# Two score passes in place of three for the second batch, one transpose in place of two

## The chip, the cores and the metric

The kernel runs on one core of one Trainium2 chip. The metric is the time in microseconds of one execution on the device; the median of several is compared. Engines are named as in the profile: PE is TensorE, PEld its weight loads, DVE is VectorE, ACT is ScalarE, POOL is GpSimd, SP is SyncE, which here only starts DMAs.

## The reference

```python
# attention: B=2, H=8, S=768, D=64, n_sink=4, window=128
scores = q @ k.T / sqrt(D)
keep = (key < 4) | ((query - key >= 0) & (query - key < 128))
a = softmax(where(keep, scores, -1e9))           # denominators + 1e-9
x = concat_heads(a @ v)                          # (2, 768, 512)
# first mixer
u = x + (x.T @ U @ V).T                          # U (768, 32), V (32, 768)
x = u + relu(u @ w_ch1) @ w_ch2                  # 512 -> 2048 -> 512
# second mixer
u = x + (relu(x.T @ w_tok1) @ w_tok2).T          # 768 -> 256 -> 768
out = u + relu(u @ w_ch1) @ w_ch2                # 512 -> 1536 -> 512
```

## The kernel before

**Number format.** Matrices are multiplied in float32r, TensorE's faster form of float32 with fewer bits. To keep precision each operand is split into a high part (the rounded value) and a low part (the rest), and a product is made of three matmul passes: high by high, high by low, low by high. ScalarE or VectorE writes high parts, VectorE or GpSimd subtracts to get low ones (`w_lo = w_raw - w_hi`, line 786).

**Attention.** Queries are cut into 12 tiles of 128 (`T`, six a batch); a head of a tile is a unit `u = 8 T + h`, from 0 to 95. The window of 128 means that a tile needs only its own keys and those of the tile before, besides the 4 sinks: 264 columns of scores, two blocks of 132. Three key tiles are kept in `k_hi` and `k_lo`. The array's 128 rows hold two heads of 64 channels. Each head's keys stand in its own half of the rows with zeros in the other half, so that the queries of a pair of heads can be the weights of both.

A unit goes as follows. TensorE makes the three score passes (L1264). VectorE adds the mask and takes the minimum of the negated scores (L1012). ScalarE makes the exponentials `probs` and their sum (L839). GpSimd copies the sink columns, already weighted, to `p_sink` (L751). TensorE transposes the two 128x128 blocks of probabilities (L1272, float32) into the bank `tp_banks`, which it shares with the transposes of q and k (L1249). ScalarE (odd units) or VectorE (even units) copies them to `probs_T` (L848, L1023). TensorE multiplies with v (L1292, float32, which the trace shows as two records a block). In a tile's last unit the sinks are transposed and multiplied (L1280, L1301), and VectorE scales the sum into `x_nat` (L1037).

In the window of a tile, own keys are kept for key <= query, those of the tile before for key > query. So the two blocks' kept entries never lie at the same place. The masked ones are zeros after the exponential.

**The plan.** One list of steps, `plan`, is built up front; every engine walks it and issues its own part of each step, in this order. Waits are semaphores. The first batch's attention runs alone, a head after the other. The second batch's (units 48 to 95) is strewn between the products of the first batch's first mixer: after every `mm1` (12 matmuls, L1413) or `mm2` (9 matmuls, L1448) one unit follows. There the transposes of unit u stand in unit u+2 and its product with v in unit u+3. Transposes of the next tile's q come in the unit h = 0, those of k and the split of q in h = 3, the splits of k (`ksplit`, `ksplit_odd`) in h = 5 and h = 7. In the first batch they stand at h = 0, 2, 4 and 6, and the lags are 2 and 4.

ScalarE copies q and k out of the bank into `q_full`, `k_full` (L815, L822), VectorE makes `q_hi` and `k_hi` (L972, L990), GpSimd `q_lo` and `k_lo` (L511, L522).

**Weights.** Each of mm1, mm2 uses one chunk of 128x512. SP loads it up to 6 ahead, ScalarE writes `w_hi` (L807) and GpSimd `w_lo` (L786) for the third chunk ahead, into rings of 4.

**The other places that the change touches.** The step `up` of layer 1, batch 0 leaves its result in four banks. ScalarE and VectorE split it into `uT_hi`, `uT_lo` (L795, L952), a quarter `kk` for each. mm1 with f = 0 begins with a wait for the last quarter, and its 12 matmuls take the quarters in turn, three each.

After this the other three mixers (layer 1 batch 1, layer 2 batches 0 and 1) use seven products of half size in place of eight (`s1`, `s2`, L1229), whose sums VectorE builds out of banks (L1132, L1135, L1138) and of which ScalarE copies the first (L924). Before each, the operands' sums are split on ScalarE (L903) and VectorE (`b_lo`, L1106). At the end of an `mm2` series in layer 2, VectorE copies the three finished output tiles to `o_stage` (L1182), and SP stores them.

## Time and profile before

| | us |
|---|---|
| median of 3 runs | 646.53 (646.51 to 646.6) |
| the profiled execution | 646.83 |
| its span, first to last instruction | 645.0 |
| TensorE busy | 628.4 (97%) |
| VectorE, ScalarE, GpSimd busy | 344.2, 323.0, 371.7 |

The profile is of one execution. Matmuls are pipelined: their records overlap, so what a matmul costs in a stream is the distance from its start to the next one's, not its duration. The first batch's attention ends at about 73 us; the units of the second lie between 73 and 237 us; the last three mixers follow.

### The profile page before, as it was taken

The numbers are of one execution on the slowest core, as the hardware profiler recorded it, in microseconds if no ns is written. First come the engines' busy times: TensorE is split into PE (matmuls) and PEld (weight loads), VectorE is DVE, ScalarE is ACT, GpSimd is POOL, SyncE is SP. The second block draws the span as 40 slices with busy tenths as digits, with TensorE's granted clock in tenths as the row PEclk, the third lists the DMA queues.
The fourth block names the chain that finished last, engine by engine and source line by source line (L and its number), as shares of the span: only waits on it lengthen the run. The fifth ranks groups of instructions, "written<-read, shape, count | busy, mean of one in ns | idle before, by whom it ended". The sixth has DMA issues, their size and how long they took to land.

```text
span 645.0 us, 10417 instructions
## 1 busy us (share of the span) xinstructions
PE 628.4 (97%) x3554; PEld 566.7 (88%) x3554; DVE 344.2 (53%) x728; ACT 323.0 (50%) x731; POOL 371.7 (58%) x371
## 2 busy tenths in 40 slices
PE   7999899999999999999999999999999999999997
PEld 6889698999999997999999988899998888899986
DVE  7776643332343336675775741396578227675411
ACT  5657655545454455745444444555444446444321
POOL 8545456655656475467566554676656446567262
PEclk9999999999999999999999999999999999999999
DMA  7434343442333324322323342433323343431142
GB/s 171 117 85 121 79 115 94 126 125 82 99 100 112 117 68 145 99 99 66 115 82 81 100 121 76 113 102 97 91 91 113 100 144 84 138 93 33 50 145 83
DMA packets 88468, 65.61 MB, mean 102 GB/s; under 512 B 43040, under 2 KB 72480, under 8 KB 88416
## 3 DMA queue, kind: packets, MB, share of 16 engines
q1 hardware_dynamic: 88416, 64.95, 35.6%
q8 instruction: 29, 0.48, 0.3%
q14 instruction: 23, 0.19, 0.1%
HBM read 61.52 MB, written 3.15 MB: 100 GB/s over the span
## 4 chain that ended last, share of the span: by engine, by line
PE 86%; DVE 7%; ACT 2%; issue 2%; POOL 1%; DMA 0%; DVEq 0%; ACTq 0%; POOLq 0%
PE bank L1448 32%; PE bank L1229 22%; PE bank L1413 10%; PE bank L1292 4%; PE bank L1264 4%; PE bank L1377 3%; PE bank L1272 3%; PE bank L1339 3%; PE bank L1249 1%; DVE b_lo L1106 1%; PE bank L1353 1%; PE bank L1320 1%; PE bank L1440 1%; DVE masked L1012 1%; POOL w_lo L786 1%
## 5 line engine op out<-in xcount | busy, mean ns | idle before, releaser
L786 POOL TENSOR_TENSOR w_lo<-w_raw,w_hi 128x512 fp32r<-128x512 f32 (+1 forms) x158 | 209.6, 1332 | 154.1 <-ACT w_hi L807 153.6
L807 ACT ACTIVATE w_hi<-w_raw 128x512 fp32r<-128x512 f32 (+1 forms) x158 | 96.8, 618 | 55.1 <-PE bank L1448 37.1
L1229 PE MATMUL bank<-b_hi,a_hi 128*128 128x384 f32 x280 | 94.7, 338 | 1.6 <-DVE temps L1135 1.5
L1229 PE MATMUL bank<-b_lo,a_hi 128*128 128x384 f32 x280 | 94.8, 338 | 0.0
L1448 PE MATMUL bank<-w_hi,hid_hi 128*128 128x512 f32 x216 | 86.8, 402 | 0.3 <-DVE hid_lo L949 0.3
L1448 PE MATMUL bank<-w_hi,hid_lo 128*128 128x512 f32 x216 | 85.1, 394 | 0.0
L1448 PE MATMUL bank<-w_lo,hid_hi 128*128 128x512 f32 x216 | 84.7, 392 | 0.0
L839 ACT ACTIVATE probs<-masked,neg_max 128x264 f32<-128x264 f32 x96 | 49.5, 516 | 69.8 <-DVE neg_max L1012 69.1
L1448 PE MATMUL bank<-w_hi,y_hid 128*128 128x512 f32 x216 | 71.1, 394 | 0.2
L1012 DVE CUSTOM_DVE_ANT_0 masked<-bank,masks 128x264 f32<-128x264 f32 x96 | 41.1, 430 | 40.0 <-PE bank L1264 36.8
L751 POOL COPY p_sink<-probs 128x12 f32<-128x12 f32 x96 | 20.3, 213 | 70.2 <-ACT probs L839 68.7
L1229 PEld LDWEIGHTS bank<-b_hi,a_hi 128*128 128x128 f32 x280 | 52.6, 188 | 3.7 <-issue 1.8
L1229 PEld LDWEIGHTS bank<-b_lo,a_hi 128*128 128x128 f32 x280 | 52.7, 188 | 1.6
L1292 PE MATMUL bank<-v_nat,probs_T 128*128 128x64 f32 x352 | 50.3, 261 | 1.3 <-DVE probs_T L1023 1.0
L949 DVE SCALAR_TENSOR_TENSOR hid_lo<-bank,hid_hi 128x384 fp32r<-128x384 f32 x32 | 17.8, 557 | 62.0 <-ACT hid_hi L795 62.0
L1292 PEld LDWEIGHTS bank<-v_nat,probs_T 128*128 128x128 f32 x352 | 48.1, 190 | 3.1 <-DVE probs_T L1023 1.4
L1448 PEld LDWEIGHTS bank<-w_hi,y_hid 128*128 128x128 f32 x216 | 40.5, 188 | 9.5 <-POOL w_lo L786 1.5
L1448 PEld LDWEIGHTS bank<-w_hi,hid_lo 128*128 128x128 f32 x216 | 40.5, 188 | 9.0
L1229 PE MATMUL bank<-b_hi,a_lo_even 128*128 128x384 f32 x140 | 47.3, 338 | 0.0
L1229 PE MATMUL bank<-b_hi,a_lo_odd 128*128 128x384 f32 x140 | 47.1, 336 | 0.0
L1413 PE MATMUL bank<-uT_hi,w_hi 128*128 128x384 f32 x128 | 45.3, 354 | 1.6 <-DVE uT_lo L952 1.6
L1448 PEld LDWEIGHTS bank<-w_hi,hid_hi 128*128 128x128 f32 x216 | 40.6, 188 | 7.0 <-issue 0.7
(157 smaller groups left out, 1423.3 us busy)
## 6 DMA issues: line engine op xcount, KB each, us to landing
w_raw<-in_moe_w_ch_dram SPq DMA_DIRECT2D x144, 256.0 KB, 2.7
w_raw<-in_moe_w_ch_dram SPq DMA_DIRECT2D x20, 512.0 KB, 3.5
q_nat<-in_q_dram SPq DMA_DIRECT2D x12, 256.0 KB, 3.0
k_nat<-in_k_dram SPq DMA_DIRECT2D x12, 256.0 KB, 3.5
v_nat<-in_v_dram SPq DMA_DIRECT2D x12, 256.0 KB, 3.5
out_dram<-o_stage SPq DMA_DIRECT2D x11, 256.0 KB, 3.4
w_raw<-in_moe_w_tok_dram SPq DMA_DIRECT2D x6, 256.0 KB, 2.7
w_raw<-in_moe_w_tok_dram SPq DMA_DIRECT2D x8, 192.0 KB, 2.4
```

What stands on the lines that cost most here:

```text
L751: nc.gpsimd.tensor_copy(p_sink[:, T % 2, :].rearrange("p (c n) -> p c n", c=3)[:, :, N_SINK * h:N_SINK * (h + 1)], probs[:, u % 4, P:BLK]. ...
L786: nc.gpsimd.tensor_tensor(w_lo[:, split % NW, 0:n], w_raw[:, split % NR, 0:n], w_hi[:, split % NW, 0:n].bitcast(f32), ALU.subtract) \
L807: nc.scalar.activation(w_hi[:, split % NW, 0:n], w_raw[:, split % NR, 0:n], ACT.Copy) \
L839: nc.scalar.activation(probs[:, u % 4, :], masked[:, u % 3, :], ACT.Exp, bias=neg_max[:, u % (2 * H):u % (2 * H) + 1], scale=-1.0, accum_o ...
L1012: nc.vector.tensor_tensor_reduce(out=masked[:, u % 3, :], in0=s_slots(u)[0][:, 0:NK], in1=masks[:, mask_of(T), :], scale=1.0, scalar=3.0e3 ...
L1229: last = mm(bank[:, 0:HALF], w[at % 2][:, a, k, :], u[:, b_part, k, :], start=(first and n == 0), stop=(n == 5), skip_group_check=True)
L1264: last = mm(bank[:, 0:NK], qs[:, T % 2, h // 2, :], keys(ks, T, h // 2, h % 2), start=(n == 0), stop=(n == 2))
L1272: last = nc.tensor.transpose(tp_banks[tp_bank_of[s]][:, j * P:(j + 1) * P], probs[:, u % 4, col:col + P], ident[:, :])
L1292: last = mm(o_bank(T)[:, h * D:(h + 1) * D], probs_T[:, u % 2, j * P:(j + 1) * P], v_nat[:, tile % 3, h * D:(h + 1) * D], start=(h == 0 an ...
L1339: last = mm(m_tile(use)[:, :], w[:, slot, cols], x[:, t % 2, :], start=(t == 0 and n == 0), stop=(t == NQ - 1 and n == 2), skip_group_chec ...
L1413: last = mm(m_tile(use)[:, 0:HALF], w[:, slot, rows], u[:, kk, cols], start=(n == 0), stop=(n == 3 * KD - 1))
L1448: last = mm(m_tile(use)[:, :], stationary, w[:, slot, :], start=False, stop=(final and n == 2), skip_group_check=True)
```

## The change

1. **Scores of the second batch (T >= 6) in two passes.** A new tile `q_both` holds, for head e of a pair, the low queries in the head's own half of the rows and its high queries in the other half. `k_hi` now holds the head's high keys in both halves, where one half was zero. One pass over `q_both` and `k_hi` gives low by high plus high by high. The second is high by `k_lo`, whose other half is still zero.
2. **What fills them.** VectorE copies the high queries to the other half (two operations of 64 rows, `q_moved`), GpSimd makes the low ones in two operations of 64 rows in place of one of 128, ScalarE copies the high keys to the other half (two operations of 64 rows, `k_moved`), and the sinks' columns once (`ksinks`).
3. **One transpose (T >= 7, 40 units).** GpSimd adds the second block of probabilities to the first. TensorE transposes the one sum. VectorE multiplies the transposed sum with two triangles of ones and gets both blocks of `probs_T`, for odd units too. The triangles are built once on GpSimd, in `o_stage`, at the step `("pv", 8)`.
4. **Output tiles of layer 2, batch 0, second half** are copied to `o_stage` by ScalarE in place of VectorE.
5. **mm1 with f = 0** waits for the quarters of `up` one after the other, each ahead of its three matmuls.
6. One buffer's name and place in memory change (`a_hi_odd` stands where a 32-column filler was).

```diff
@@ blocks
+            if T > NQ:
+                return [(0, T), (0, T - 1)]
@@ query_low(eng, wait, T)
+            if T >= NQ:
+                for e in range(2):
+                    rows = slice(e * D, (e + 1) * D)
+                    wait(q_split, queries_split(T - 1) + e)
+                    eng.tensor_tensor(q_both[rows, T % 2, :, e, :], q_full[rows],
+                                      q_hi[rows, T % 2, :, :].bitcast(f32), ALU.subtract).then_inc(q_split, 1)
+                wait(q_split, queries_split(T))
+                return
@@
+        def two_triangles(T):
+            return T > NQ
         def by_act(u):
-            return u % 2 == 1
+            return u % 2 == 1 and not two_triangles(u // H)
+        def copied_by_act(s):
+            return s[:4] == ("mm2", 2, 0, 1)
@@ gpsimd, scores
+                    if two_triangles(T):
+                        pool.wait_ge(probs_ready, u + 1)
+                        nc.gpsimd.tensor_tensor(probs[:, u % 4, 0:P], probs[:, u % 4, 0:P],
+                                                probs[:, u % 4, BLK:BLK + P], ALU.add).then_inc(blocks_added, 1)
@@ gpsimd, qsplit
                     pool.wait_ge(q_high, s[1] + 1)
+                    pool.wait_ge(psink_ready, copied)
+                    if split:
+                        pool.wait_ge(wlo_ready, split)
@@ gpsimd
+                elif s == ("pv", H):
+                    nc.gpsimd.memset(triangles[:, :, :], 1.0).then_inc(triangles_built, 1)
...
@@ scalar
+                elif s[0] == "ksplit" and s[1] >= NQ:
+                    T = s[1]
+                    act.wait_ge(k_copied, T + 1)
+                    act.wait_ge(scores_ready, H * (T - 1))
+                    for e in range(2):
+                        src = list(key_parts(k_hi, T))[e][0]
+                        last = nc.scalar.activation(k_hi[(1 - e) * D:(2 - e) * D, :, e, T % 3, 0:P], src, ACT.Copy)
+                    last.then_inc(k_moved, 1)
...
@@ scalar, sinksT
+                    if two_triangles(T):
+                        wait_drained(act, ("probsT", H * T + H - 1))
@@ scalar
+                elif copied_by_act(s) and ends(s):
+                    for i in range(TPH):
+                        act.wait_ge(m_ready, m_at[s[:4], i] + 1)
+                        act.wait_ge(out_stored[i], 16)
+                        nc.scalar.activation(o_stage[:, i, :], m_tile((s[:4], i))[:, :], ACT.Copy).then_inc(y_copied, 1)
@@ vector, qsplit
+                    if T >= NQ:
+                        for e in range(2):
+                            rows, there = slice(e * D, (e + 1) * D), slice((1 - e) * D, (2 - e) * D)
+                            moved = nc.vector.tensor_copy(q_both[there, T % 2, :, e, :], q_full[rows])
+                        moved.then_inc(q_moved, 1)
@@ vector, probsT
+                    if two_triangles(u // H):
+                        dve.wait_ge(triangles_built, 3)
+                        nc.vector.tensor_tensor(probs_T[:, u % 2, :].rearrange("p (a b) -> p a b", a=2),
+                                                transposed[:, 0:P].unsqueeze(1).broadcast_to([P, 2, P]),
+                                                triangles[:, :, :], ALU.mult).then_inc(probsT_by_dve, 1)
@@ tensor, scores
-                    for n, (qs, ks) in enumerate(((q_hi, k_hi), (q_hi, k_lo), (q_lo, k_hi))):
+                    if T < NQ:
+                        passes = ((high, k_hi), (high, k_lo), (low, k_hi))
+                    else:
+                        passes = ((q_both[:, T % 2, h // 2, h % 2, :], k_hi), (high, k_lo))
@@ tensor, probsT
                     pe.wait_ge(probs_ready, u + 1)
                     tp_free(s)
+                    if two_triangles(u // H):
+                        pe.wait_ge(blocks_added, u - (NQ + 1) * H + 1)
@@ tensor, mm1
-                    if f == 0:
-                        wait_out((("up", layer, b, half), KD - 1))
...
                     for kk in range(KD):
                         rows = slice(kk * P, (kk + 1) * P)
+                        if f == 0:
+                            wait_out((("up", layer, b, half), kk))
```

## Rows read from the trace of the kernel before

**Rows 1.** The page: busy time, share and instructions; the chain by engine.
```profile
PE 628.4 (97%) x3554; PEld 566.7 (88%) x3554; DVE 344.2 (53%) x728; ACT 323.0 (50%) x731; POOL 371.7 (58%) x371
...
PE 86%; DVE 7%; ACT 2%; issue 2%; POOL 1%; DMA 0%; DVEq 0%; ACTq 0%; POOLq 0%
```

**Rows 2.** Windows: stretch, its length, busy us of each engine, granted clock, DMA.
```profile
79.00:91.00 12.00, 10.14 (x62) 9.28 (x61) 6.28 (x19) 6.88 (x18) 4.83 (x7) 1.00 0.50 136
...
130.00:157.00 27.00, 26.85 (x172) 24.90 (x172) 8.99 (x30) 13.53 (x36) 16.33 (x20) 1.00 0.39 108
```

**Rows 3.** Timeline of one unit: start us, duration us, engine, instruction.
```profile
182.94 0.28 PE L1264 MATMUL bank<-k_hi,q_hi 128*128 128x264 f32 x1
...
183.18 0.29 PE L1264 MATMUL bank<-k_hi,q_lo 128*128 128x264 f32 x1
...
183.30 0.55 PE L1292 MATMUL bank<-v_nat,probs_T 128*128 128x64 f32 x4
...
183.69 0.39 PE L1272 MATMUL bank<-ident,probs 128*128 128x128 f32 x2
...
183.92 0.27 PE L1280 MATMUL bank<-ident,p_sink 128*96 128x128 f32 x1
...
184.65 0.19 POOL L751 COPY p_sink<-probs 128x12 f32<-128x12 f32 x1 [1.32 <-ACT probs L839]
```

**Rows 4.** Timeline of a unit that begins with the transposes of k.
```profile
163.74 0.60 ACT L822 ACTIVATE uT_full<-bank 128x512 f32<-128x512 f32 x1 [1.24 <-PE bank L1249]
...
163.84 0.55 PE L1292 MATMUL bank<-v_nat,probs_T 128*128 128x64 f32 x4
...
164.48 0.41 PE L1272 MATMUL bank<-ident,probs 128*128 128x128 f32 x2
```

**Rows 5.** Timeline ahead of the first mm1.
```profile
78.87 1.95 DVE L952 TENSOR_TENSOR uT_lo<-bank,uT_hi 128x384 fp32r<-128x384 f32 x4 [1.05 <-ACT uT_hi L795]
...
80.88 0.44 PE L1413 MATMUL bank<-uT_hi,w_hi 128*128 128x384 f32 x1 [1.56 <-DVE uT_lo L952]
...
81.09 0.29 DVE L1023 COPY probs_T<-bank 128x128 f32<-128x128 f32 x1
```

**Rows 6.** Timeline of the last mixer's first products.
```profile
542.36 1.14 ACT L807 ACTIVATE w_hi<-w_raw 128x512 fp32r<-128x512 f32 x2
...
543.05 3.50 POOL L786 TENSOR_TENSOR w_lo<-w_raw,w_hi 128x512 fp32r<-128x512 f32 x2 [0.45 <-ACT w_hi L807]
...
547.28 1.87 DVE L1182 COPY o_stage<-bank 128x512 f32<-128x512 f32 x3
...
548.53 0.33 PE L1229 MATMUL bank<-b_hi,a_lo_even 128*128 128x384 f32 x1
...
549.65 0.56 DVE L1135 TENSOR_TENSOR temps<-bank,temps 128x384 f32<-128x384 f32 x1
...
550.36 0.41 PE L1229 MATMUL bank<-b_hi,a_hi 128*128 128x384 f32 x1 [1.50 <-DVE temps L1135]
```

**Rows 7.** Groups by form, whole span: count, busy us, mean ns of one, idle before.
```profile
L786 POOL TENSOR_TENSOR w_lo<-w_raw,w_hi 128x512 fp32r<-128x512 f32 x150 | 201.5, 1348 | 144.0 <-ACT w_hi L807 143.6
...
L522 POOL TENSOR_TENSOR k_lo<-uT_full,k_hi 64x512 fp32r<-64x512 f32 x22 | 28.4, 1291 | 6.2 <-DVE k_hi L990 2.4 <-POOL w_lo L786 2.0 <-POOL p_sink L751 0.3
...
L1023 DVE COPY probs_T<-bank 128x256 f32<-128x256 f32 x40 | 16.9, 422 | 7.6 <-PE bank L1272 7.3
...
L511 POOL TENSOR_TENSOR q_lo<-uT_full,q_hi 128x512 fp32r<-128x512 f32 x11 | 14.1, 1282 | 2.7 <-DVE q_hi L972 2.7
...
L990 DVE CAST k_hi<-uT_full 64x512 fp32r<-64x512 f32 x22 | 11.0, 498 | 0.2
...
L786 POOL TENSOR_TENSOR w_lo<-w_raw,w_hi 128x384 fp32r<-128x384 f32 x8 | 8.2, 1035 | 10.0 <-ACT w_hi L807 10.0
```

**Rows 8.** Timeline: ScalarE where tile 6 is prepared, VectorE's casts of tile 7.
```profile
65.18 0.52 ACT L839 ACTIVATE probs<-masked,neg_max 128x264 f32<-128x264 f32 x1 [0.72 <-DVE neg_max L1012]
...
90.46 1.84 DVE L990 CAST k_hi<-uT_full 64x512 fp32r<-64x512 f32 x2
```

More of the change, by code:

```diff
@@ L362, in attention_then_two_mixers @@
         temps = sb("temps", [P, 3, HALF])
-        sb("above_probs", [P, 32])
+        a_hi_odd = sb("a_hi_odd", [P, 7, 2, P], f32r)
         w1_sums = sb("w1_sums", [P, 3, 2, P])
         w1_raw = sb("w1_raw", [P, 2, KD, 2 * P])
-        a_hi = [sb(f"a_hi{i}", [P, 7, 2, P], f32r) for i in range(2)]
+        a_hi = [sb("a_hi_even", [P, 7, 2, P], f32r), a_hi_odd]
         a_lo = [sb("a_lo_even", [P, 7, 2, P], f32r), a_lo_odd]
@@ L507, in by_pair, with queries_split, query_low @@
             return bank[:, :].rearrange("p (a b) -> p a b", a=PAIRS)
-        def query_low(eng, T):
+        def queries_split(T):
+            return T + 1 if T < NQ else 2 * (T + 1) - NQ
+        def query_low(eng, wait, T):
+            if T >= NQ:
[6 more added lines that the diff above has]
+                return
             eng.tensor_tensor(q_lo[:, T % 2, :, :], q_full,
@@ L540, in o_bank, with act_copies @@
             return o_banks[T % 2] if T < NQ else o_banks[0]
+        def two_triangles(T):
+            return T > NQ
         def by_act(u):
-            return u % 2 == 1
+            return u % 2 == 1 and not two_triangles(u // H)
+        def act_copies(u):
+            return sum(by_act(v) for v in range(u + 1))
         def wait_drained(eng, s):
@@ L584, in attention_then_two_mixers @@
         for key in m_at:
-            if y1_at(key) is None and not (key[0][0] == "up" and key[0][1:3] in SEVEN):
+            if y1_at(key) is None and not copied_by_act(key[0]) and not (key[0][0] == "up" and key[0][1:3] in SEVEN):
                 drained_at[key] = len(drained_at)
@@ L1166, in _ @@
                     low_of((s, 0), every, hid_lo[:, hid_slot(s), :], hid_hi[:, hid_slot(s), :], relu=True)
+                elif copied_by_act(s):
+                    stored += TPH if ends(s) else 0
                 elif s[0] == "mm2" and ends(s):
@@ L1262, in _ @@
                         pe.wait_ge(masked_ready, u - n + 1)
-                    for n, (qs, ks) in enumerate(((q_hi, k_hi), (q_hi, k_lo), (q_lo, k_hi))):
-                        last = mm(bank[:, 0:NK], qs[:, T % 2, h // 2, :], keys(ks, T, h // 2, h % 2),
-                                  start=(n == 0), stop=(n == 2))
+                    high, low = q_hi[:, T % 2, h // 2, :], q_lo[:, T % 2, h // 2, :]
+                    if T < NQ:
+                        passes = ((high, k_hi), (high, k_lo), (low, k_hi))
+                    else:
+                        passes = ((q_both[:, T % 2, h // 2, h % 2, :], k_hi), (high, k_lo))
+                    for n, (queries, ks) in enumerate(passes):
+                        last = mm(bank[:, 0:NK], queries, keys(ks, T, h // 2, h % 2),
+                                  start=(n == 0), stop=(n == len(passes) - 1))
                     last.then_inc(scores_ready, 1)
@@ L1270, in _ @@
                     tp_free(s)
-                    for j, (col, _) in enumerate(blocks(u // H)):
+                    if two_triangles(u // H):
+                        pe.wait_ge(blocks_added, u - (NQ + 1) * H + 1)
+                    for j, (col, _) in enumerate(blocks(u // H)[0:1 if two_triangles(u // H) else 2]):
                         last = nc.tensor.transpose(tp_banks[tp_bank_of[s]][:, j * P:(j + 1) * P],
```

56 lines of the change are left out of this document (44 added, 12 removed).

## The prediction

> **What bounds the kernel now.** I read the page first: TensorE is busy 97% of the span, and 86% of the chain that ended last is its work [rows 1]. A busy share can hide stalls, so I next cut the changed stretch, from 79 us (where the second batch's heads lie between the first mixer's products) to 233 us, into windows. From 130 to 157 us, eight heads, TensorE is busy 26.85 of 27 at a granted clock of 1.00 (2.4 GHz), while VectorE, ScalarE and GpSimd have 9.0, 13.5 and 16.3 us of work. Only the first window, 79 to 91 us, has a hole, 10.14 of 12 [rows 2]. So work taken from TensorE there shortens the span, as long as nobody else falls behind. Last I read the timeline at one head and at the two places where other edits lie.
>
> **The score passes.** One head's first pass starts at 182.94, its third at 183.18, the next work at 183.30 [rows 3]: 0.12 us a pass. One pass goes in each of 48 heads: 48 x 0.12 = 5.8 us. The pass over stacked rows has the same shape as the one it replaces, so it costs the same. The Trainium skill (TensorE: Matmul & The Clock Gate, Back-to-back issue gap) gives N/2.4 + 2.5 ns, 112 ns here, an estimate by which this term is 5.4; the row decides.
>
> **The transposes.** For tiles 7 to 11 (40 heads) one of two goes. Two start at 183.69 and the next transpose, of the same length, at 183.92 [rows 3]: 0.115 each. 40 x 0.115 = 4.6, and with the change of kind behind them nearer 4.8, which I take; bounds 4.6 and 5.2 (0.13 each). The same page and section has about 81 ns a matmul at N = 128 in a stream, an estimate of 3.2 us for this term; these are float32 transposes and the trace is slower than that, so the trace's number stands.
>
> **What the shorter head gives back.** Where a head begins with the transposes of q or k, the next probability transpose needs the same bank, which ScalarE first has to copy out. At 163.74 ScalarE copies for 0.60, TensorE's four p.v matmuls start at 163.84 and the transpose at 164.48 [rows 4]. The four take 0.39 elsewhere (183.30 to 183.69) [rows 3], so 0.25 us are a wait. It hangs on the copy, not on the passes, so a pass removed ahead of it only lengthens it. There are nine such heads (q for tiles 8 to 11, k for 7 to 11): -9 x 0.12 = -1.1 us.
>
> **The wait by quarters before the first mm1.** TensorE is idle 1.56 us until 80.88, for VectorE's four uT_lo subtractions that begin at 78.87 and take 1.95 [rows 5]. It needs only the first quarter to begin: ready at about 78.87 + 0.55 = 79.4. A quarter's three matmuls last 0.53, a subtraction 0.49, so each later quarter is ready when wanted. Start at 79.5 instead of 80.88: 1.4, less a little for breaking the stream of weight loads: 1.3 us. What is next late is the bank of the following k transposes, which holds until VectorE has copied out head 48's probabilities at 81.4 [rows 5]; the product now ends near 81.7, so it just fits. Bounds: 0.7 (if this and the tile's masks bite) to 1.4. The same edit at the second half finds its quarters long drained: nothing.
>
> **The output copies moved to ScalarE.** At 547.28 VectorE comes from a series of b_lo subtractions to copy three output tiles (1.87 us), and only then makes the next mixer's sums, the second at 549.65; TensorE stands 1.50 idle until 550.36 for it [rows 6]. Without the copies the two sums (0.56 each) run from 547.4 to 548.5. TensorE's last matmul before the hole begins at 548.53 and the next one would begin 0.18 later, at 548.7: nearly all of 550.36 - 548.7 = 1.65 comes back. ScalarE takes the three copies at 0.6 each (a 128x512 copy out of a bank [rows 4]) from 543.5, when its two w_hi end [rows 6], to 545.3. Behind them is its copy of the first product, half a microsecond, which VectorE wants at 547.4. Its three a_hi come a microsecond later too, and their user GpSimd is busy with w_lo until 546.55 [rows 6]. The stores, issued on SP some steps into the next mixer, find the tiles ready as before. I take 1.6; bounds 0.8 to 1.7.
>
> **What is added, and its cover.** *GpSimd.* The add of two 128x128 blocks is not in the trace. Its two-input operation takes 1348 ns for 512 columns and 1035 for 384 [rows 7], 2.45 ns a column, which leaves 0.41 us for 128. From below it is bounded by the 12-column p_sink copy, 0.19 [rows 3], from above by the full 512-column operation, 1.35. I take 0.41, which the slope of two rows supports. The q_lo of a tile becomes two operations on half the rows; k_lo shows that half the rows cost the same, 1291 against 1282 ns [rows 7]: +1.29 us a tile. In 130 to 157 us GpSimd was busy 16.33 of 27 [rows 2]; it becomes 16.33 + 1.29 + 8 x 0.41 = 20.9, in 27 - 8 x 0.24 = 25.1. It stays under. Behind the add on its queue are p_sink, then w_lo for the third chunk ahead, which has some two steps of 3 us in hand, and the next tile's q_lo and k_lo. TensorE now waits for the add: probabilities of a head are ready about 1.7 us after its passes begin (182.94 to the p_sink copy at 184.65 [rows 3]), and their transpose comes two heads later, some 6 us after. Even behind two q_lo's (2.6) and a w_lo (1.3) the add keeps the date. Cost 0; if that cover goes, see the rivals.
> *VectorE.* The product with the triangles replaces a copy out of the same bank, 422 ns [rows 7], and has as many columns; it may cost up to the 384-column sum out of a bank, 0.56 [rows 6]. It takes over ScalarE's 20 copies. With the two q moves (0.50 each, as its k_hi cast [rows 7]) that is 4 x 0.42 + 1.0 = 2.7 us more in a tile, at most 4.3, on 9 of 27 busy [rows 2]. Hidden; what waits behind is the mask of the head, which TensorE wants only at the next head's passes, 3 us on.
> *ScalarE.* Two k moves of at most 0.6 in (half the rows of the copy in [rows 4]), four copies of some 0.4 out: even.
> *At the border of the batches* cover is thinner, since heads follow each other in 1.2 us. Tile 6's preparation adds 1.2 us to ScalarE just ahead of a probability that runs at 65.18 after 0.72 idle [rows 8]: that one comes half a microsecond late, and is used four heads on. GpSimd gets a second q_lo there and, in the first batch, the triangles (three small operations, together under one q_lo); head 48 waits for two small moves more. I charge 0.4 for all of this; bounds 0 and, if each of the two ScalarE moves and the q_lo comes through, 2.5.
>
> **Sum.** 5.8 + 4.8 - 1.1 + 1.3 + 1.6 - 0.4 = 12.0 us. The profiled execution took 646.83; the span is 645.0, with 1.8 around it, unchanged. 646.83 - 12.0 = 634.8. The median before, 646.53, is 0.3 lower than that execution, so the median should be about 634.5, which I predict.
>
> **Rivals.**
> *A, only removed matmuls pay.* The 1.56 and 1.50 us holes move instead of closing: head 48's bank and masks are late after the first, the b_lo series rules after the second. For it: both are chains through VectorE, and 81.4 against 81.7 is close. Against: in both the next thing is ready by the rows. Time: 646.5 - (5.8 + 4.8 - 1.1 - 0.4) = 637.4.
> *B, GpSimd late in some heads.* Its two-input operations stretch when VectorE works beside: two w_lo's took 3.50 beside b_lo [rows 6], and two k_hi casts 1.84 in place of 1.0 [rows 8]. New VectorE moves come exactly when the two q_lo's run. If the transposes of the three heads a tile with q_lo or k_lo work (15) wait 0.3 us each, that is 4.5 back: 639. The Trainium skill (GPSIMD Engine Reference, Engine selection) says to put elementwise two-input work on VectorE and not here, and in Key points that the two share SBUF interfaces; the stretched rows agree with the sharing. Against: over 3 us of slack.
> *C, slower: GpSimd becomes the bound.* Between tiles 7 and 11 every head needs its add. From an add of (25.1 - 17.6)/8 = 0.94 us on, GpSimd has no idle time and sets the pace; at 1.35, the price of the full 512 columns, eight heads take 17.6 + 10.8 = 28.4 instead of 27: 5 x 1.4 = 7 us lost, against 2.9 gained at the two holes and 1 in tile 6: 650. For it: half the rows cost as much as all, so size isn't everything here. Against: the slope over columns.
> *D, the passes pay less than their spacing*, because a hidden limit (weight loads are busy 24.9 of 27 us [rows 2]) steps in: half of 10.6 less: 640.
>
> **How the numbers follow.** Forecast 0.73, A 0.12, B 0.07, C 0.03, D 0.05. Added bounds of the terms put the forecast between 646.5 - (5.8 + 5.2 - 1.1 + 1.4 + 1.7) = 633.5 and 646.5 - (5.8 + 4.6 - 1.1 + 0.7 + 0.8 - 2.5) = 638.2; A's 637.4 lies inside. The range is 632.9 to 638.6: it leaves B, C and D out, and takes in that half of the 1.1 is not given back. What can be told from no change is about 0.2%, 1.3 us: faster 0.95, same 0.02, slower 0.03, of which the slower is C.
>
> **What would show it.** Right: 48 score passes and 40 transposes fewer; heads 0.24 us shorter; the first mm1 starting near 79.5; no hole of over 0.3 us among the first products of the last mixer; an add of some 0.4 us; GpSimd near 83% in the middle windows. Wrong: TensorE idle until the add at a transpose (B, C), a hole of the same size moved a few matmuls on (A), or passes spaced wider than 0.12 us (D).

## The result, and the profile after

The changed kernel takes **638.50 us** (median of 4 runs, 638.29 to 638.59) against 646.57 (646.51 to 646.72) for the kernel before, run beside it: ratio 0.9874, 95% interval 0.9857 to 0.9892. That is 8.1 us faster where 12.0 had been forecast, and 0.1 inside the upper end of the range (638.6). The profiled execution took 638.47, of which the span is 636.4.

What an execution takes beyond its span isn't the same for all kernels: 1.8 us for the kernel before, 2.1 for the changed one and for e1, e5 and e7 below, 1.7 for e4 and e12, and it varies by about 1 us between executions of e6 and of e8. The profile doesn't say what it is. So the medians of two kernels can lie 0.3 to 0.4 us closer or further apart than their spans.

The page of the kernel after, the lines that answer to [rows 1]: 88 matmuls fewer, as many as the change takes out.

```profile
PE 619.0 (97%) x3466; PEld 556.3 (87%) x3466; DVE 360.0 (57%) x757; ACT 326.5 (51%) x728; POOL 396.8 (62%) x420
...
PE 85%; DVE 8%; issue 3%; ACT 2%; POOL 1%; DMA 0%; DVEq 0%; ACTq 0%; POOLq 0%
```

TensorE's busy time fell by 9.4 us (628.4 to 619.0), the span by 8.6. The same windows as [rows 2]:

```profile
79.00:91.00 12.00, 10.23 (x59) 8.94 (x60) 7.67 (x18) 6.33 (x18) 6.75 (x7) 1.00 0.51 132
130.00:157.00 27.00, 26.65 (x167) 24.64 (x166) 14.73 (x40) 14.88 (x39) 21.27 (x31) 1.00 0.45 120
```

In the middle of the tiles it went as forecast: TensorE nearly full, GpSimd at 21.3 of 27 us. In the first window it did not: of the 1.56 us hole of [rows 5] 0.39 is left, and TensorE has still as little work done, 10.23 of 12. Something else opened there. VectorE got more work than the bound allowed. The products take 0.42 in each of a tile's eight heads in place of four, and the two q moves take 3.0: 4.7 us more in a tile in the middle, where "at most 4.3" stood, a bound whose terms the text doesn't give.

The groups of instructions between 79 and 233 us, by form (count, busy us, mean ns of one, idle before), show the price of what was added:

```profile
L786 POOL TENSOR_TENSOR probs<-probs 128x128 f32<-128x128 f32 x40 | 19.4, 484 | 21.3 <-ACT probs L908 19.7 <-POOL q_both L528 0.4
L1108 DVE TENSOR_TENSOR probs_T<-bank,o_stage 128x256 f32<-128x256 f32 x40 | 16.8, 421 | 2.5 <-PE bank L1374 1.1 <-PE bank L1382 0.5
...
L1052 DVE CAST q_both<-uT_full 64x512 fp32r<-64x512 f32 x10 | 12.8, 1276 | 0.2
```

The add takes 0.48 us (0.41 was taken), the product with the triangles 0.42 (as taken). A q move on VectorE takes 1.28 us where 0.50 had been taken.

**How to find where time went.** For two kernels with the same order of work I subtract the start of the same matmul: the second score pass (k_lo, q_hi) of each head, and the first product with b_hi, a_hi of each step of the mixers. I call the difference the lead over before. Heads are counted from 0; head 48 is the first of tile 6. The leads, in us, of the kernels that the text below needs most (e9, e10 and so on are the names of the runs below):

| lead at | head 50 | 51 | 53 | 55 | 95 | mixer (1,1) begins | last mixer, before its sums | after them | last product |
|---|---|---|---|---|---|---|---|---|---|
| after | -0.97 | +0.36 | -1.23 | -1.01 | 6.27 | 5.69 | 6.58 | 8.42 | 8.66 |
| only the transposes (e4) | -0.24 | 1.09 | 0.96 | 0.96 | 4.77 | 5.10 | 5.97 | 7.81 | 8.05 |
| q moves on ScalarE (e9) | -1.08 | 0.25 | 0.23 | -0.53 | 6.19 | 5.61 | 6.22 | 8.01 | 8.25 |
| q, k transposes inside (e10) | -0.69 | 0.34 | -1.16 | -0.95 | 7.46 | 6.88 | 7.71 | 9.48 | 9.72 |
| both of these (e11) | -0.83 | 0.19 | 0.42 | -0.35 | 8.43 | 7.85 | 8.46 | 10.26 | 10.49 |
| only the transposes, inside (e12) | -0.14 | 0.91 | 1.01 | 1.02 | 5.99 | 6.31 | 7.14 | 8.91 | 9.15 |

In the row "after" 0.7 us are lost at the border of the batches, ahead of head 50 (0.26 of the -0.97 is there from the start of the kernel). The quarter wait gives 1.33 at head 51; 1.6 us are lost again by head 53; then 7.3 us come in over the 40 heads from 55 to 95; 0.6 are lost before the mixer (1,1); 1.8 come at the last mixer's sums.

**Where the 1.6 us went** is seen in the timeline of the kernel after, 84 to 90 us:

```profile
84.97 1.84 DVE L1052 CAST q_both<-uT_full 64x512 fp32r<-64x512 f32 x2
...
85.02 2.94 POOL L528 TENSOR_TENSOR q_both<-uT_full,q_hi 64x512 fp32r<-64x512 f32 x2 [0.36 <-DVE q_hi L1048]
...
86.85 0.43 DVE L1093 CUSTOM_DVE_ANT_0 masked<-bank,masks 128x264 f32<-128x264 f32 x1
...
87.32 0.52 ACT L908 ACTIVATE probs<-masked,neg_max 128x264 f32<-128x264 f32 x1 [3.16 <-DVE neg_max L1093]
...
87.84 0.26 ACT L917 ACTIVATE probs_T<-bank 128x128 f32<-128x128 f32 x1
87.99 0.48 ACT L846 ACTIVATE uT_hi<-bank 128x384 fp32r<-128x384 f32 x1
...
88.15 0.43 PE L1394 MATMUL bank<-v_nat,probs_T 128*128 128x64 f32 x2 [0.29 <-ACT probs_T L917]
...
88.50 0.56 DVE L1028 TENSOR_TENSOR uT_lo<-bank,uT_hi 128x384 fp32r<-128x384 f32 x1 [1.22 <-ACT uT_hi L846]
...
89.12 0.55 PE L1455 MATMUL bank<-ident,x_nat 128*128 128x128 f32 x3 [0.42 <-DVE uT_lo L1028]
```

Start at 88.15. TensorE waits there for probabilities that ScalarE copied at 87.84. Their transpose was done since 84.6; but in ScalarE's order the copy stands behind the exponential of the next head (87.32), which waits for VectorE's mask (86.85), which stands behind the two q moves (84.97). So a move that TensorE needs 16 us later (tile 7's first pass starts at 101.26) delays by 1.8 us a copy that is needed now. ScalarE was idle 3.16 us ahead of it.

The larger wait is one link further down the same queue. Behind the copy ScalarE splits `uT_hi` (87.99), from it VectorE makes `uT_lo` (88.50), and TensorE waits for that at 89.12. From the product with v to these next transposes it is 0.97 us, where it was 0.28 before. The late mask itself shifts the score passes of head 52 by another 0.3.

**The border of the batches**, in the timeline from 62 to 69 us: the q moves of tile 6 (0.43 each here), then VectorE's k_hi casts of the same tile, ScalarE's new k moves, and who waits.

```profile
62.76 0.86 DVE L1052 CAST q_both<-uT_full 64x512 fp32r<-64x512 f32 x2
...
65.59 1.26 DVE L1071 CAST k_hi<-uT_full 64x512 fp32r<-64x512 f32 x2
...
66.61 1.27 ACT L891 ACTIVATE k_hi<-uT_full 64x512 fp32r<-64x512 f32 x2
...
67.48 0.69 DVE L1125 TENSOR_TENSOR x_nat<-bank,recip 128x512 f32<-128x512 f32 x1
...
68.23 0.67 PE L1422 MATMUL bank<-x_nat,U_sb 128*96 128x512 f32 x1 [0.70 <-DVE x_nat L1125]
```

VectorE is late with the tile's output: before, its q_hi cast ended at 62.46 with 0.65 us to spare before the mask, the k_hi casts took 0.85 and not 1.26, and TensorE waited 0.14 us for x_nat; now it waits 0.70.

**A new hole of 0.91 us behind the heads**, in the timeline from 226 to 241 us:

```profile
226.97 0.46 POOL L786 TENSOR_TENSOR probs<-probs 128x128 f32<-128x128 f32 x1 [0.63 <-ACT probs L908]
...
233.07 5.05 POOL L837 TENSOR_TENSOR w_lo<-w_raw,w_hi 128x512 fp32r<-128x512 f32 x4
...
236.85 1.43 DVE L1143 TENSOR_TENSOR b_hi<-U_sb,b_hi 128x128 fp32r<-128x128 f32 x1 [0.44 <-ACT b_hi L936]
...
238.34 2.38 DVE L1148 TENSOR_TENSOR b_lo<-x_nat,b_hi 128x512 fp32r<-128x512 f32 x2
...
238.63 1.53 POOL L837 TENSOR_TENSOR w_lo<-w_raw,w_hi 128x512 fp32r<-128x512 f32 x1 [0.51 <-ACT w_hi L858]
...
240.86 0.47 PE L1415 MATMUL bank<-b_hi 128*128 128x512 f32 x1 [0.91 <-DVE b_lo L1148]
```

The same two b_lo took 1.28 us in the kernel before. Here GpSimd's w_lo begins ahead of the second one, and they take 2.38. The lead falls from 6.73 at the first product with these operands to 5.69 behind them: 1.0 us. The change doesn't touch these operations; e6 below shows what shifted them.

**The last mixer**, the answer to [rows 6]. ScalarE copies the tiles at 536.82, VectorE goes from its b_lo straight to the sums, and the stream of products has no hole as in [rows 6]:

```profile
536.82 1.55 ACT L994 ACTIVATE o_stage<-bank 128x512 f32<-128x512 f32 x3
...
540.70 0.55 DVE L1220 TENSOR_TENSOR temps<-bank,temps 128x384 f32<-128x384 f32 x1
541.28 0.56 DVE L1223 TENSOR_TENSOR temps<-bank,temps 128x384 f32<-128x384 f32 x1
```

### The profile page after: what moved, and what is told of

Same layout as the page of the kernel before. It is cut to its first block, busy times and chain, and to the rows that moved or that the text cites. A ratio compares the mean times of both kernels' runs of the same rounds, so it can differ in the third digit from the quotient of the medians.

```text
span 636.4 us, 10351 instructions
## 1 busy us (share of the span) xinstructions
PE 619.0 (97%) x3466; PEld 556.3 (87%) x3466; DVE 360.0 (57%) x757; ACT 326.5 (51%) x728; POOL 396.8 (62%) x420
## 4 chain that ended last, share of the span: by engine, by line
PE 85%; DVE 8%; issue 3%; ACT 2%; POOL 1%; DMA 0%; DVEq 0%; ACTq 0%; POOLq 0%
PE bank L1550 33%; PE bank L1321 23%; PE bank L1515 9%; PE bank L1394 4%; PE bank L1364 3%; PE bank L1479 3%; PE bank L1441 3%; PE bank L1374 2%; PE bank L1341 1%; DVE b_lo L1194 1%; PE bank L1455 1%; DVE masked L1093 1%; PE bank L1422 1%; PE bank L1542 1%; DVE b_lo L1148 1%
## 5 line engine op out<-in xcount | busy, mean ns | idle before, releaser
L1321 PE MATMUL bank<-b_hi,a_hi_even 128*128 128x384 f32 x140 | 47.1, 336 | 0.1
L1321 PE MATMUL bank<-b_hi,a_hi_odd 128*128 128x384 f32 x140 | 46.9, 335 | 0.0
L1321 PE MATMUL bank<-b_lo,a_hi_odd 128*128 128x384 f32 x140 | 46.9, 335 | 0.0
L1321 PE MATMUL bank<-b_lo,a_hi_even 128*128 128x384 f32 x140 | 46.9, 335 | 0.0
L1550 PEld LDWEIGHTS bank<-w_lo,hid_hi 128*128 128x128 f32 x216 | 40.6, 188 | 6.7
```

The costliest lines, as they stand in the source:

```text
L1321: last = mm(bank[:, 0:HALF], w[at % 2][:, a, k, :], u[:, b_part, k, :], start=(first and n == 0), stop=(n == 5), skip_group_check=True)
L1550: last = mm(m_tile(use)[:, :], stationary, w[:, slot, :], start=False, stop=(final and n == 2), skip_group_check=True)
```

## The experiments

All were timed beside the kernel before. The theory that I had formed from the traces (M in the expectations): each part pays what it was said to pay where it stands, and the missing 4 us are handed back at places where VectorE or ScalarE, not TensorE, sets the pace. Its rivals: H, a shift of the engines against each other accounts for the loss; D, the passes pay less than their spacing; B, GpSimd is late. From e9 on the rival is R: work taken from one late engine only makes the next one late.

### One wait in place of four (e1)

```diff
+                    if f == 0:
+                        wait_out((("up", layer, b, half), KD - 1))
...
-                        if f == 0:
-                            wait_out((("up", layer, b, half), kk))
```

> The changed kernel, with the first mm1 waiting once, for the last quarter, as before the change. Theory M (late masks: VectorE's moves of q hold the mask of head 51 back, and with it the probabilities, and that chain begins only when mm1 has ended, so it follows mm1 wherever it lies): the 1.3 us that the quarters brought are lost again, 639.8. Rival H (the hole only moved: mm1 ends too early for what follows it, and heads 52 and 53 pay 1.6 us for that): nothing changes, 638.3 to 638.6.

Measured 639.29 (638.99 to 640.31), ratio 0.9885 (0.9872 to 0.9899). That lies between M's 639.8 and H's 638.6 at most. The hole is back:

```profile
81.55 0.44 PE L1515 MATMUL bank<-uT_hi,w_hi 128*128 128x384 f32 x1 [1.69 <-DVE uT_lo L1028]
```

Its lead at head 50 is -0.68 where after has -0.97: 0.29 that the two have apart since their first microseconds. Beyond that it is 1.33 behind after at head 51, 0.75 at head 53, and 1.04 at the end (lead 7.91); the medians differ by 0.8. So the wait by quarters gains 1.3 where it stands, as forecast. By head 53 0.6 of it is handed back, and at the end 0.3; the medians say 0.5.

### The output copies on VectorE again (e2)

```diff
-            return s[:4] == ("mm2", 2, 0, 1)
+            return False
```

> The changed kernel, with the output tiles of layer 2, batch 0, second half copied by VectorE again. In the changed trace the hole of 1.5 us is gone; both theories expect it back: 638.5 + 1.6 = 640.1. Should other work take its place, 638.5.

Measured 641.13 (640.25 to 641.97), ratio 0.9906 (0.9891 to 0.9921). The lead behind the sums is 6.47 in place of 8.42: this part is worth 1.95 us there, where 1.6 had been expected. The medians are 2.6 apart, and the four executions are spread over 1.7 us. In the profiled one another 1.1 us lie behind the last product (4.9 us to the end of the span, 3.8 in after), where the output is stored; nothing here tells why. The timeline has the sequence of [rows 6] again:

```profile
540.85 1.87 DVE L1272 COPY o_stage<-bank 128x512 f32<-128x512 f32 x3
...
543.93 0.41 PE L1321 MATMUL bank<-b_hi,a_hi_even 128*128 128x384 f32 x1 [1.50 <-DVE temps L1223]
```

### The two halves of the change alone (e3, e4)

e3, two transposes again, passes as changed:

```diff
-            return T > NQ
+            return False
...
-            if T > NQ:
-                return [(0, T), (0, T - 1)]
```

> The changed kernel with two transposes a head and no add and no triangle product in tiles 7 to 11 (score passes stay two). Theory M: 40 transposes come back at 0.12 us each, 638.5 + 4.8 = 643.3; ScalarE has its 20 copies again, and they stand behind exponentials that late masks delay, which costs up to 1 us more. Rival D (removed matmuls pay half their spacing): 638.5 + 2.4 = 640.9.

Measured 643.26 (642.4 to 643.54), ratio 0.9941 (0.9929 to 0.9954). M had 643.3. Its lead at the last product is 3.99, so taking one transpose in place of two is worth 4.7 us on top of the passes, near the forecast. But other things are mixed into this number. Over heads 55 to 95 after gains 5.3 us on e3, more than the transposes' own spacing gives (37 of them, 0.115 each: 4.3), because e3 has ScalarE copy probabilities again, and these copies stand behind the exponentials that the q moves delay:

```profile
115.32 0.66 PE L1392 MATMUL bank<-v_nat,probs_T 128*128 128x64 f32 x4 [0.26 <-ACT probs_T L915]
```

Behind the heads after loses 1.0 of it in the b_lo hole, which e3 doesn't have.

e4, one transpose, three passes as before, nothing held twice:

```diff
-                        if T >= NQ:
-                            pe.wait_ge(q_moved, T - NQ + 1)
-                            pe.wait_ge(k_moved, T - NQ + 2)
...
-                    if T < NQ:
+                    if True:
                         passes = ((high, k_hi), (high, k_lo), (low, k_hi))
```

(with all moves and the second q_lo left out)

> The changed kernel with three score passes and without all that fills the stacked rows (no moves of q and k, one q_lo of 128 rows); transposes stay one a head. Theory M: +5.8 us of passes, -0.7 us at the border and -1.6 us at heads 52 and 53, which the preparation causes: 642.0. Rival D: passes pay half, +2.9 - 2.3: 639.1. Rival H: preparation costs nothing at heads 52 and 53, +5.8 - 0.7: 643.6.

Measured **638.61** (638.38 to 638.99), ratio 0.9873 (0.9859 to 0.9886): as fast as the whole change. M had 642.0, H 643.6; D's 639.1 is the closest (e5 answers it). The half of the change that stands first in its name, 48 passes fewer, is worth next to nothing on balance: 0.1 us by the medians, 0.6 by the leads. Row "only the transposes" of the table says where it went. By head 55 it leads after by 1.97, though it has run seven passes more (0.84): the preparation costs 2.8. Over the next 40 heads after gains 3.5 on it, where 40 x 0.12 are 4.8: another 1.3 gone. And it has no b_lo hole (1.0). 5.8 - 2.8 - 1.3 - 1.0 leaves 0.7; the leads at the end differ by 0.6.

### The third pass back, the preparation kept (e5)

```diff
-                        passes = ((q_both[:, T % 2, h // 2, h % 2, :], k_hi), (high, k_lo))
+                        passes = ((q_both[:, T % 2, h // 2, h % 2, :], k_hi), (high, k_lo), (high, k_lo))
```

It adds one product twice; only the time counts.

> The changed kernel with the second score pass of the second batch made twice, so that TensorE has its 48 passes back while all preparation stays as changed (the scores come out wrong by one low term; only the time is read). Theory M: 48 x 0.12 = 5.8 us less what the nine heads with q or k transposes swallow, 1.1: 643.2. Rival D (a pass pays half its spacing): 641.1.

Measured 641.44 (641.18 to 641.75), ratio 0.9916 (0.9901 to 0.9932). M had 643.2, D 641.1. 48 passes cost 2.9 us here, not 5.8. The leads divide it: up to head 55 they cost 0.4 of 0.84, over heads 55 to 95 3.5 of 4.8 (the rest falls into waits), and the b_lo hole isn't there, which gives 1.0 back. D's number is close, its mechanism isn't there: in after the passes of a head stand at 95.12 and 95.24, the next work at 95.36, and the lead grows by 0.22 to 0.24 a head wherever no wait follows.

### No add on GpSimd (e6)

The add of the two probability blocks and TensorE's wait for it are left out, so half of each window is missing from the output; only the time counts.

```diff
-                    if two_triangles(T):
-                        pool.wait_ge(probs_ready, u + 1)
-                        nc.gpsimd.tensor_tensor(probs[:, u % 4, 0:P], probs[:, u % 4, 0:P],
-                                                probs[:, u % 4, BLK:BLK + P], ALU.add).then_inc(blocks_added, 1)
```

> The changed kernel without GpSimd's add and without the wait for it: the first block of probabilities alone is transposed (attention over half the window; only the time is read). Theory M: the add is never waited for, 638.5, or 0.2 less since GpSimd leaves VectorE's moves more room. Rival B (GpSimd late): up to 2 us faster, 636.5.

Measured 637.79 (637.22 to 638.61), ratio 0.9856 (0.9835 to 0.9877). M had 638.5 or 0.2 less, B 636.5. In the heads the leads are those of after within 0.2; TensorE never waited for the add. What it gains, 0.7 by the medians and 0.9 by the leads, comes at one place: the b_lo hole isn't there.

```profile
236.93 1.01 DVE L1139 TENSOR_TENSOR b_hi<-U_sb,b_hi 128x128 fp32r<-128x128 f32 x1 [0.44 <-ACT b_hi L932]
...
238.00 1.28 DVE L1144 TENSOR_TENSOR b_lo<-x_nat,b_hi 128x512 fp32r<-128x512 f32 x2
...
238.72 1.71 POOL L833 TENSOR_TENSOR w_lo<-w_raw,w_hi 128x512 fp32r<-128x512 f32 x1 [0.93 <-ACT w_hi L854]
```

The two traces, laid over each other at the first product with b_hi (239.32 in after, 239.40 in e6), show the steps. In after the last head's add (226.97) stands ahead of GpSimd's weight work, which then runs without a pause and ends 1.20 us before that product (238.12). In e6 it ends 1.61 before (237.79). VectorE's b_hi subtraction runs beside it and takes 1.43 us in place of 1.01, so VectorE's second b_lo starts 0.4 later. In e6 it starts 0.1 ahead of GpSimd's next w_lo and takes 0.68; in after 0.3 behind it, and takes 1.78. The next w_lo itself starts 0.69 before the product in both. The traces of all kernels agree: the hole is in the eight that have both the add and two passes (after, e1, e2, e7 to e11) and in none of the six that lack one or both (before, e3 to e6, e12). So B falls for the heads, but GpSimd is late by 0.4 us at their end, and that, through VectorE, costs 1.0.

### The q moves elsewhere (e7, e8, e9)

If the q moves at 84.97 are the cause, they must be put where nobody waits. Three tries. e7, still on VectorE, in the same head of the tile before as in after, but behind its mask and not ahead of it:

```diff
+                    if NQ <= N < NTILES and u % H == (2 if T < NQ else 3):
+                        for e in range(2):
+                            ...
+                            moved = nc.vector.tensor_copy(q_both[there, N % 2, :, e, :], q_full[rows])
```

> The changed kernel with VectorE's two q moves behind the mask of the same head in place of ahead of it. Theory M: the late masks go, and with them most of the 0.7 us at the border and of the 1.6 us at heads 52 and 53: 636.7. The moves still take up to 3 us a tile beside GpSimd, so what stands behind them on VectorE (the copy of probabilities) is late instead, hence not all. Rival H: 638.5.

Measured 640.70 (640.61 to 640.98), ratio 0.9905 (0.989 to 0.992): 2.2 slower than after, where M had 636.7. Timeline and windows at the border of the batches:

```profile
63.68 2.54 DVE L1097 CAST q_both<-uT_full 64x512 fp32r<-64x512 f32 x2
66.14 0.41 DVE L1113 COPY probs_T<-bank 128x256 f32<-128x256 f32 x1
...
66.70 0.41 PE L1375 MATMUL bank<-ident,probs 128*128 128x128 f32 x2 [1.89 <-DVE probs_T L1113]
```

```profile
64.00:68.00 4.00, 2.11 (x17) 1.92 (x15) 3.91 (x8) 1.17 (x7) 2.13 (x3) 0.94 0.86 195
68.00:72.00 4.00, 4.00 (x20) 3.46 (x20) 2.03 (x8) 3.06 (x8) 2.73 (x5) 0.64 0.01 4
```

The two casts took 2.54 in place of 0.86, and TensorE stood 1.89 idle; behind that its granted clock is 0.64 of full on average over 4 us. At heads 52 and 53 the mask is no longer late, but 1.15 us are lost all the same (1.59 in after): the two moves take 2.70 us at 87.75, and now `uT_lo` stands behind them.

e8, the q moves and the k moves on ScalarE, behind exponentials of the tile before:

```diff
+                    if NQ <= N < NTILES and h == (3 if T < NQ else 4):
+                        ...
+                            last = nc.scalar.activation(q_both[there, N % 2, :, e, :], q_full[rows], ACT.Copy)
+                    if NQ <= N < NTILES and h == (4 if T < NQ else 5):
+                        ...
+                            last = nc.scalar.activation(k_hi[(1 - e) * D:(2 - e) * D, :, e, N % 3, 0:P], src, ACT.Copy)
```

> The changed kernel with the q moves on ScalarE, behind an exponential one head later, and the k moves behind that head's exponential too. Theory M: ScalarE does not share GpSimd's way to the memory, a move takes 0.63 us there, and no mask waits: the whole 2.3 us come back, 636.2. Rival H: 638.5 less 0.7 at the border, 637.8.

Measured 640.74 (639.9 to 641.54), ratio 0.9905 (0.9889 to 0.9922), where M had 636.2. The gain and a new loss both happened. The lead at head 53 is +0.30 in place of -1.23: the 1.5 us came back. Then the k moves did two heads later what the q moves had done, on the other engine:

```profile
94.55 1.27 ACT L916 ACTIVATE k_hi<-uT_full 64x512 fp32r<-64x512 f32 x2
95.72 0.26 ACT L924 ACTIVATE probs_T<-bank 128x128 f32<-128x128 f32 x1
...
96.03 0.43 PE L1396 MATMUL bank<-v_nat,probs_T 128*128 128x64 f32 x2 [1.58 <-ACT probs_T L924]
...
98.43 0.63 PE L1552 MATMUL bank<-w_hi,hid_hi 128*128 128x512 f32 x1
98.86 0.63 PE L1552 MATMUL bank<-w_lo,hid_hi 128*128 128x512 f32 x1
```

The matmuls of 512 columns follow each other in 0.43 us instead of 0.23 until 99.7. This trace is of the slowest of the five executions (641.54, mean clock 0.997). Another has 0.997 too; the three others have a mean clock of 1.00 and spans of 637.9 to 638.2, 1.5 to 1.8 above after's. So the hole costs about its own length, and the slow stretch behind it comes in some executions only.

e9, only the q moves on ScalarE; the k moves stay:

> The q moves on ScalarE, two heads ahead of the tile, as in the run before; the k moves stay where the change has them. M (the two casts of the q move on VectorE, 1.84 us beside GpSimd's q_lo at 84.97, are what hands back the gain at head 52; and the hole of 1.58 us at 96.03 in the run before came from the k moves, that stood ahead of ScalarE's copy of the probabilities): the 1.5 us of head 52 come back and the hole doesn't: 637.0 (636.6 to 637.6). R (the work is only pushed to the next late engine): 638.2 to 638.8, with a new wait behind the exponential that the moves now follow.

Measured 638.50 (638.09 to 638.62), ratio 0.9868 (0.9853 to 0.9883). At head 53 the lead is +0.23, 1.46 more than after, and the chain is as M has it:

```profile
84.97 0.42 DVE L1096 CUSTOM_DVE_ANT_0 masked<-bank,masks 128x264 f32<-128x264 f32 x1
...
87.42 0.33 PE L1397 MATMUL bank<-v_nat,probs_T 128*128 128x64 f32 x2
```

But the time is that of after; M had 637.0, R 638.2 to 638.8. Of the 1.46 us, 0.98 are gone at head 55 (the tile's k_hi casts, 1.85 us, now come in time to be waited for: 0.18 for a mask, 0.29 for ScalarE's copy), 0.3 at head 57 (the wait for uT_full grows from 0.45 to 0.72), 0.5 at head 86; some 0.35 come back between. M is right about the cause at head 52, and R about what it is worth.

### The q and k transposes inside the product ahead (e10), and with the q moves on ScalarE (e11)

The wait named under "what the shorter head gives back" is [rows 4] again; in after, the timeline of the same unit:

```profile
160.95 0.60 PE L1341 MATMUL bank<-ident,k_nat 128*128 128x128 f32 x4
...
161.63 0.55 PE L1394 MATMUL bank<-v_nat,probs_T 128*128 128x64 f32 x4
...
161.67 0.60 ACT L877 ACTIVATE uT_full<-bank 128x512 f32<-128x512 f32 x1 [1.04 <-PE bank L1341]
...
162.37 0.30 PE L1374 MATMUL bank<-ident,probs 128*128 128x128 f32 x1 [0.18 <-issue]
162.51 0.41 PE L1515 MATMUL bank<-uT_hi,w_hi 128*128 128x384 f32 x1
```

From k's transposes to the probability transpose it is 1.42 us (1.44 before) though a pass less lies between. The edit moves the transposes and ScalarE's copy forward:

```diff
+                        if kk == 2 and s in next_tp:
+                            nat_transposes(next_tp[s])
...
+                        if i == 1 and s in next_tp:
+                            nat_transposes(next_tp[s])
... (scalar)
+                if s in next_tp:
+                    copy_nat(next_tp[s])
```

> The transposes of a tile's queries and keys, and ScalarE's copies of them, are put inside the product of the first batch ahead of them, ahead of its last third, in place of behind it. M (at the nine heads with such transposes the shorter passes only lengthen the wait for ScalarE's uT_full copy, 0.3 to 0.6 us each): the copy is under way before the probabilities are asked for: 9 x 0.3 to 0.4 = 3 us: 635.5 (634.8 to 636.5). R (the wait is for ScalarE's queue, and other copies come late instead): 638 to 639.

Measured 637.59 (637.4 to 638.53), ratio 0.986 (0.9843 to 0.9876). M had 635.5, R 638 to 639. A gain of 0.9, of which the heads behind q's transposes (57, 65, 73, 81) show 0.4 to 0.5 each. At those behind k's the 0.4 to 0.6 gained (60, 68, 76) are lost one head earlier (0.6 to 0.7 at 59, 67, 75), where TensorE now waits for VectorE to leave the bank, and another 0.5 goes from head 84 to 87:

```profile
158.92 0.41 DVE L1119 TENSOR_TENSOR probs_T<-bank,o_stage 128x256 f32<-128x256 f32 x1
...
159.48 0.63 PE L1348 MATMUL bank<-ident,k_nat 128*128 128x128 f32 x4 [0.38 <-DVE probs_T L1119]
```

> Both edits of the two runs ahead. If their gains are independent, their sum: 638.5 - 1.5 - 3.0 = 634.0. If one eats the other: the better of the two, 635.5.

Measured **636.49** (636.26 to 636.56), ratio 0.9837 (0.9823 to 0.9852): the fastest, 2.0 under after. The q moves on ScalarE, worth nothing alone, are worth 1.1 us on top of e10 by the medians and 0.8 by the leads. M's sum had 634.0 or, if one eats the other, 635.5.

### Only the transposes, with those inside (e12)

e4 and e10 together.

> The transposes' half of the change alone (three passes, no moves, as in the earlier run of 638.61), with the q and k transposes inside the product ahead. M (the passes' 5.8 us are eaten in part by the wait at those heads, in part by the moves and the b_lo split): with neither of these in the way the passes are worth what is left over; this kernel keeps the wait-free heads but not the passes: 638.6 less 9 x 0.2 = 636.8, so that the kernel with both edits beats it by 2.8 us. R (the score passes' half is worth nothing however it is prepared): as fast as the kernel with both edits, within 0.6 us.

Measured 637.49 (637.3 to 637.62), ratio 0.9853 (0.9838 to 0.9868). Against e11 it is 1.0 us slower by the medians, 1.3 by the leads. So the score passes' half of the change is worth 1.0 to 1.3 us when it is prepared better, and 0.1 to 0.6 as it was made: neither 2.8 (M) nor nothing (R, within 0.6).

## Why the prediction was right, and where it was not

The sign, the order of size and most terms held; one term, the cover of the added work, was wrong by 2.4 us, and one loss wasn't in the sum. That the range still holds the result is luck. The added bounds of the terms end at 638.2, and 638.50 lies beyond them; it lies within the range only by the 0.4 us between 638.2 and 638.6, for which the text gives no term. From the leads:

| term | forecast | measured | from |
|---|---|---|---|
| 48 passes | +5.8 | +5.8 gross | 0.12 apart |
| given back at the heads with q or k transposes | -1.1 | -1.3 | passes only: after against e4, heads 55 to 95, 3.5 in place of 4.8 |
| border, q moves, second q_lo | -0.4 | -2.8 | after against e4, up to head 55 |
| b_lo beside w_lo | none | -1.0 | after: 6.73 to 5.69; e3 to e6 and e12 don't have it |
| transposes | +4.8 | +4.1 | e4: head 55 to the first b_hi product, 0.96 to 5.10 |
| quarter wait | +1.3 | +1.2 | e4, heads 50 to 53 |
| output copies | +1.6 | +1.8 | after; 1.95 by e2 |
| in no term: start of the kernel, stretches from mixer (1,1) on | none | +0.9 | -0.26, then 0.9 and 0.24 |
| sum | 12.0 | 8.7 | span: 8.6 |

The terms are differences between kernels, and they depend on each other: against e3 the transposes come out at 4.7, against the kernel before at 4.1 (e4).

**The passes and the transposes** are sized rightly by their spacing: the lead grows by 0.23 a head where no wait follows. For the transposes the estimate of 3.2 us from the Trainium skill (TensorE: Matmul & The Clock Gate, Back-to-back issue gap) would have been further off.

**What the shorter head gives back** is the mechanism forecast. It takes the gain of the removed transpose too: at heads 65, 68, 73, 76, 81 and 84 the lead grows by 0.04 to 0.08, where 0.12 had been left to them (the one transpose at 162.37 takes 0.14 to the next work, as the two at 164.48 did within 0.02). Nine heads alone would make 1.4 to 1.8 of both halves; what is booked here is what the passes lose.

**The preparation is the step that failed.** The text said of VectorE "with the two q moves (0.50 each, as its k_hi cast)", "Hidden; what waits behind is the mask of the head, which TensorE wants only at the next head's passes, 3 us on", and charged 0.4 at the border. Two errors. The size: a k_hi cast's mean of 498 ns [rows 7] mixes some 0.42 alone, for most of the 22, with 1.42 for the one that ran beside GpSimd, the second of the 1.84 pair in [rows 8]; and the q moves are placed where GpSimd's q_lo runs, in all tiles but the first of them. The larger one is the chain: behind the mask stands the exponential, and behind that, on ScalarE's queue, a copy of probabilities that TensorE wants at once. I asked who waits for the mask and not what is queued behind those who wait for it. e9 shows the chain: with the q moves off VectorE the 1.5 us at heads 52 and 53 come back. It also shows that the chain isn't the only thing in the way, since other waits take them again. The bound of 2.5 was given for the border of the batches alone, and 2.8 is more; 0.7 of it lies at the border, the rest at heads 48 to 55. Rival B named the collision (new VectorE moves beside two q_lo) but looked for the loss on GpSimd.

**The quarter wait** was right, 1.3; the order "the product now just fits" too. But the first product starts at 80.55 and not near 79.5, since TensorE comes there 0.97 late; less that it is 79.58. In the whole change a part of it is handed back by head 53 (e1), since there a wait on VectorE stands next.

**GpSimd** is at 79% in 130 to 157 us (83% forecast), the add takes 0.48 (0.41 forecast), and no transpose waits for it: C is out, and B as it was written. GpSimd's delay of 0.4 us at the end of the heads (e6) is of B's kind, at a place that neither the sum nor B had. **A** is out by e2 and e1: both holes pay when they close. Its number, 637.4, is nearer to the result than the forecast's. **D**'s halved spacing is nowhere in the rows.

**What stays open**: the lead grows by 0.8 to 0.9 us between mixer (1,1) and the last mixer (0.6 in e8, e9 and e11, where TensorE waits 0.34 for a w_lo near 398 us), and by 0.24 behind it in every variant, mostly in steps of a hundredth per product. No row is large enough to name the cause. The medians, 8.1 apart, are 0.5 closer than the spans, of which 0.3 is time beyond the span.

## What to carry to other kernels

For work put on a side engine, price it in the company that it will have, and follow each queue two steps: the instruction behind it, the one that waits for that, and what stands behind that one on its own queue. Removing matmuls pays in full only where no other engine's date comes next; where a copy or a cast sets the date, first move that. And test the halves of a change apart: here one half carried nearly all of the gain, and the other paid 1 us only when two further edits, one of them worth nothing alone, had cleared its way. A range that is wider than its terms add up to should say which term the rest belongs to.

## What the runs showed of the hardware

A 64x512 cast from SBUF to SBUF on VectorE took 0.43 us alone (62.76, two in 0.86) and 1.52 beside GpSimd's two-input operations (two in 3.04, timeline of after):

```profile
161.00 3.04 DVE L1052 CAST q_both<-uT_full 64x512 fp32r<-64x512 f32 x2
```

In these pairs it mattered who began first: the pair at 84.97, begun 0.05 ahead of GpSimd's q_lo, took 1.84 (0.42 and 1.41), the pair at 161.00, begun 0.03 behind a w_lo, 3.04. On ScalarE the same move took 0.63 in each of the twelve cases of e11. VectorE's operations out of a bank kept their 0.42 (probs_T 421 ns mean) in the same stretch. The Trainium skill (GPSIMD Engine Reference, 1. Specifications) has VectorE contend with GpSimd for SBUF when it is in a two-port mode or reads two SBUF inputs. The b_lo, with two SBUF inputs, agree (0.68 alone, 1.78 beside w_lo). The casts read one input and contend too; that they are in a two-port mode no run here shows. The factor of 3.5 is the trace's.

A hole of 1.58 us in e8 and one of 1.89 in e7 were followed by matmuls at about half their pace for some 3.5 us, granted clock 0.74 and 0.64 in the 4 us windows behind, the lower of the two levels, 1.2 GHz, for most of it. Behind e1's hole of 1.69 us and before's of 1.56 the clock stayed at 1.00 in such windows, so the length of the hole alone doesn't tell the cases apart. In e7 all five executions have a mean clock below 1.00 (0.996 or 0.997), in e8 two of five. In e8 head 55 is 3.3 us later against head 54 than in before, twice the hole of 1.58; in e7 head 45 is 2.6 later than in after, 0.7 more than its hole. The windows of e8:

```profile
94.00:98.00 4.00, 2.42 (x11) 2.02 (x12) 0.96 (x4) 2.97 (x8) 2.23 (x3) 0.83 0.23 66
98.00:102.00 4.00, 4.00 (x19) 3.45 (x18) 1.15 (x4) 1.99 (x6) 2.37 (x3) 0.74 0.23 66
```
